# Splitting the first expert tile inside the last dense block of a fused attention, gated feed-forward and routed-experts kernel

## What is computed

```python
state = w * state + k_t v_t^T;  y_t = r_t (state + u k_t v_t^T)      # 4 x 8 heads, 768 steps, head width 48
x = (silu(x @ w_gate) * (x @ w_val)) @ w_out                         # 384 -> 1536 -> 384, every token
e = argmax(x @ moe2_w_gate)                                          # one of 8 experts for each token
out = softmax(logits)[e] * sigmoid(x @ w_output_gate)[e] * (relu(x @ w1[e]) @ w2[e])   # 384 -> 1024 -> 384
```

## Time and profile before

| | |
|---|---|
| median of 3 runs | 907.48 us (907.06 to 910.53) |
| the profiled execution: its time | 907.18 us |
| its span, first to last instruction | 905.2 us |
| mean granted TensorE clock | 0.987 of full |
| TensorE matmul busy | 859.2 us (95% of the span) |
| VectorE busy | 586.8 us (65%) |
| ScalarE busy | 300.2 us (33%) |
| GpSimd busy | 177.6 us (20%) |

### The profile page before, as it was taken

One profiled execution on the slowest core, in us unless ns is written; L12 is line 12 of the kernel. 1 busy time (PEld: TensorE's weight loads), 2 busy tenths in 40 slices (PEclk: granted clock), 3 DMA queues, 4 the chain that ended last, 5 costly groups with the idle time before them and its releaser, 6 DMA issues.

```text
span 905.2 us, 15624 instructions
## 1 busy us (share of the span) xinstructions
PE 859.2 (95%) x5725; PEld 762.4 (84%) x5725; DVE 586.8 (65%) x1075; ACT 300.2 (33%) x472; POOL 177.6 (20%) x146
## 2 busy tenths in 40 slices
PE   5799999999999999999999999997799999999996
PEld 5678888888888888888888888886799999999995
DVE  8778756675567555634443454486768777987781
ACT  1223223111311131113112312453337565665550
POOL 4823302332133312320100010130010101010110
PEclk9999999999999999999999999998899999999998
DMA  9743420242024201410010003355876668676700
GB/s 380 255 175 130 143 89 22 80 158 63 0 83 147 89 1 63 157 70 1 10 53 27 1 36 126 140 207 197 328 278 225 244 241 311 244 231 248 273 17 18
DMA packets 35934, 125.78 MB, mean 139 GB/s; under 512 B 4044, under 2 KB 19328, under 8 KB 30256
## 3 DMA queue, kind: packets, MB, share of 16 engines
q1 hardware_dynamic: 31504, 108.20, 34.5%
q0 software_dynamic: 3520, 9.87, 2.8%
q10 hardware_dynamic: 864, 7.08, 2.1%
HBM read 107.32 MB, written 18.88 MB: 139 GB/s over the span
## 4 chain that ended last, share of the span: by engine, by line
PE 84%; DVE 5%; issue 3%; DMA 3%; SPq 1%; ACT 1%; POOL 1%; DVEq 0%; ACTq 0%; POOLq 0%
PE bank L1449 33%; PE bank L1493 6%; PE bank L1495 5%; PE bank L1494 5%; PE bank L1608 4%; PE bank L1610 3%; PE bank L1609 3%; PE bank L1590 3%; PE bank L1591 3%; PE bank L1592 3%; PE bank L1374 3%; PE bank L1394 3%; PE bank L1587 2%; PE bank L1359 2%; PE bank L1386 2%
## 5 line engine op out<-in xcount | busy, mean ns | idle before, releaser
L1449 PE MATMUL bank<-X1H,WH 128*128 128x512 f32 x432 | 169.5, 392 | 4.3 <-DVE X1L L999 4.3
L1449 PE MATMUL bank<-X1H,WL 128*128 128x512 f32 x432 | 168.7, 391 | 0.0
L1449 PE MATMUL bank<-X1L,WH 128*128 128x512 f32 x432 | 168.7, 390 | 0.0
L1095 DVE TENSOR_TENSOR TT<-bank,SG 128x512 f32<-128x512 f32 x72 | 49.8, 691 | 125.0 <-ACT SG L755 124.6
L755 ACT ACTIVATE SG<-bank 128x512 f32<-128x512 f32 x72 | 43.1, 598 | 238.7 <-PE bank L1449 238.7
L686 ACT ACTIVATE AH<-PP 128x512 fp32r<-128x512 f32 (+1 forms) x78 | 46.2, 600 | 162.0 <-DVE PP L1100 162.0
L1449 PEld LDWEIGHTS bank<-X1H,WH 128*128 128x128 f32 x432 | 81.5, 189 | 21.1 <-issue 4.4
L1103 DVE TENSOR_TENSOR AL<-PP,AH 128x512 fp32r<-128x512 f32 (+1 forms) x78 | 63.2, 817 | 50.9 <-ACT AH L686 50.9
L1449 PEld LDWEIGHTS bank<-X1H,WL 128*128 128x128 f32 x432 | 81.4, 188 | 17.1
L1449 PEld LDWEIGHTS bank<-X1L,WH 128*128 128x128 f32 x432 | 81.5, 189 | 16.6
L1493 PE MATMUL bank<-AH,WH 128*128 128x512 f32 (+1 forms) x234 | 90.9, 389 | 0.0
(11 more groups left out here) (226 smaller groups left out, 1872.7 us busy)
## 6 DMA issues: line engine op xcount, KB each, us to landing
W_EVEN<-w SPq DMA_DIRECT2D x20, 1536.0 KB, 9.5
W_ODD<-w SPq DMA_DIRECT2D x18, 1536.0 KB, 9.2
RK_IN<-unit_rk SPq DMA_DIRECT2D x18, 736.0 KB, 5.5
V_IN<-unit_v SPq DMA_DIRECT2D x18, 448.0 KB, 3.7
STG<-w_dense ACTq DMA_DIRECT2D x6, 1152.0 KB, 5.4
X<-mixed SPq DMA_DIRECT2D x6, 768.0 KB, 4.4
mixed<-YS SPq DMA_DIRECT2D x40, 96.0 KB, 2.0
XG_ODD<-store SPq DMA_DIRECT2D x9, 394.0 KB, 8.4
```

What stands on the lines that cost most here:

```text
L1095: tt(TT[:, :], GATE_PS[:, :], SG[:, :], ALU.mult).then_inc(gate_free, 1)
L1449: last = mm(bank_[:, :], lhs[:, f, m, k * P:k * P + P], rhs[:, k, :], start=(x == 0), stop=(x == len(terms) - 1))
```

## The change

The high and low parts of tile 0's W1 and rows, and the high parts of its W2, are made inside the last dense block (W1 at f = 9 and 10, rows at f = 10 after a `turn_rows` on PE placed there, W2 highs at f = 10 and 11). The first two slices of tile 0's up product run ahead of the last down product, the others behind it. To have the PSUM banks free for that, the hidden banks are taken in the order 5, 0, 1, 6. PAD is filled in the block at f = 6, and the early tiles are chosen at f = 4 (two) and f = 5. SP loads tile 2 right behind W1 of tile 1, ahead of the pad stores. POOL's slice of W1 low is now one of tile 1, not of tile 0. The tail of the last block is put between the steps of tile 0 in a new order on each engine: on DVE the low parts of tile 1's W1 and rows and gates(0) are made ahead of positions(CH); on PE ranks(CH) and the turning of tile 1's rows are between the two halves of tile 0's down product. Functions that only moved up in the file are left out of the diff.

```diff
-        H_PS, XT_PS, YO_PS = (bank[0], bank[1], bank[5], bank[6]), (bank[7], bank[4]), bank[2:4]
+        H_PS, XT_PS, YO_PS = (bank[5], bank[0], bank[1], bank[6]), (bank[7], bank[4]), bank[2:4]
...
+            load_tile(EARLY_TILES[2], early_row(2), early_expert(2))
 
             sp.wait_ge(base_ready, 1)
+            sp.wait_ge(padding, 2)
             sp.nop(nofuse=True)
             for x in range(NE):
                 row = sp.value_load(BASEI[0:1, x:x + 1], min_val=x * REGION, max_val=x * REGION + TOK)
                 sp.dma_start(store[bass.ds(row, SLOT), :].rearrange("(a p) c -> p a c", p=P), PAD[:, :, :])\
                   .then_inc(pad_written, 16)
-            load_tile(EARLY_TILES[2], early_row(2), early_expert(2))
 
...
-            pool.wait_ge(w1_high, 2)
+            tile = EARLY_TILES[1]
+            pool.wait_ge(w1_high, 3 * tile.n + 2)
+            pool.wait_ge(w1_low, 3 * tile.n)
             cut = slice(EF, 2 * EF)
-            nc.gpsimd.tensor_tensor(W1L[0][:, cut], W1[0][:, cut], W1H[0][:, cut], ALU.subtract).then_inc(w1_low, 1)
+            nc.gpsimd.tensor_tensor(W1L[1][:, cut], W1[1][:, cut], W1H[1][:, cut], ALU.subtract).then_inc(w1_low, 1)
...
+                    if last and f == 9:
+                        w1_highs(EARLY_TILES[0])
+                    if last and f == 10:
+                        x_highs(EARLY_TILES[0])
+                        w2_highs(EARLY_TILES[0], 0)
+                    if last and f == 11:
+                        w2_highs(EARLY_TILES[0], 1)
...
-                    if isinstance(tile.n, int) and tile.n == 0:
-                        if f % 2 == 0:
-                            w2_highs(tile, f // 2)
-                    elif next_tile and f < KT:
+                    if next_tile and f < KT:
                         w1_highs(next_tile, range(f, f + 1))
                 if next_tile:
                     act.wait_ge(hidden_ready, 4 * tile.n + 4)
                     x_highs(next_tile)
-                    if isinstance(tile.n, int) and tile.n == 0:
-                        w1_highs(next_tile)
                     w2_highs(next_tile, 0)
                     w2_highs(next_tile, 1)
 
-            act.wait_ge(value_ready, FT * CH)
-            w1_highs(EARLY_TILES[0])
+            dense_block(0)
+            with act.Fori(1, CH - 1) as n:
+                dense_block(n)
+            dense_block(CH - 1)
+
+            tile, following = EARLY_TILES[0], EARLY_TILES[1]
+            hidden_highs(tile, 0)
             x2_copies(CH)
-            x_highs(EARLY_TILES[0])
+            hidden_highs(tile, 1)
             rec_copies(CH)
-            act.wait_ge(x2_ready, KT * CH)
-
-            expert_tile(EARLY_TILES[0], EARLY_TILES[1])
+            hidden_highs(tile, 2)
+            hidden_highs(tile, 3)
+            w1_highs(following)
+            exps(tile)
+            x_highs(following)
+            w2_highs(following, 0)
+            w2_highs(following, 1)
...
+            def fill_pad():
+                for x in range(2):
+                    dve.wait_ge(y_stored[x], 64 * CH - 64)
+                dve.wait_ge(r_scaled, UNITS)
+                nc.vector.memset(PAD[:, :, :], 0.0).then_inc(padding, 1)
+                dve.wait_ge(padding, 1)
+                for x in range(2):
+                    last = nc.vector.tensor_scalar(PAD[:, x, R_ID:R_ID + 1], CST[:, C_TOK:C_TOK + 1], float(TOK + x * P),
+                                                   None, ALU.add)
+                last.then_inc(padding, 1)
...
-                        if last and f in (4, 5, 6):
-                            choose_early(f - 4)
+                        if last and f == 4:
+                            choose_early(0)
+                            choose_early(1)
+                        if last and f == 5:
+                            choose_early(2)
+                        if last and f == 6:
+                            fill_pad()
+                        if last and f == 9:
+                            w1_lows(EARLY_TILES[0], (0, 1))
+                        if last and f == 10:
+                            w1_lows(EARLY_TILES[0], (2,))
+                            x_lows(EARLY_TILES[0])
...
-            for x in range(2):
-                dve.wait_ge(y_stored[x], 64 * CH - 64)
-            dve.wait_ge(r_scaled, UNITS)
-            c = Chain(setup, c.at + c.k)
-            c.step(nc.vector.memset(PAD[:, :, :], 0.0))
-            for x in range(2):
-                c.step(nc.vector.tensor_scalar(PAD[:, x, R_ID:R_ID + 1], CST[:, C_TOK:C_TOK + 1], float(TOK + x * P), None,
...
-            w1_lows(EARLY_TILES[0], (0,))
-            x2_copy(CH)
-            w1_lows(EARLY_TILES[0], (2,))
-            x_lows(EARLY_TILES[0])
-            rec_copy(CH)
-            copy_logits(CH)
-            gates(EARLY_TILES[0])
-            route(CH)
-            copy_ranks(CH)
-            positions(CH)
-            nc.vector.tensor_copy(BASEI[:, :], BASE[:, :]).then_inc(base_ready, 1)
...
-                first = isinstance(tile.n, int) and tile.n == 0
-                if not first:
-                    gates(tile)
+                gates(tile)
                 if tile.half_tile:
                     sum_halves(tile, 0)
                     sum_halves(tile, 1)
@@ -1251,23 +1259,38 @@
                     hidden_lows(tile, f)
                     if tile.half_tile and f < 2:
                         sum_halves(tile, f + 2)
-                    if first:
-                        if f % 2 == 0:
-                            w2_lows(tile, f // 2)
-                    elif next_tile and f < KT:
+                    if next_tile and f < KT:
                         w1_lows(next_tile, range(f, f + 1))
                     if isinstance(tile.n, int) and tile.n == 1:
                         (plan_counts, plan_kinds, plan_entries, plan_rows)[f](plan)
                 if next_tile:
                     x_lows(next_tile)
-                    if first:
-                        w1_lows(next_tile)
                     w2_lows(next_tile, 0)
                     w2_lows(next_tile, 1)
                 scale_rows(tile)
 
-            dve.wait_ge(x2_ready, KT * CH)
-            expert_tile(EARLY_TILES[0], EARLY_TILES[1])
+            tile, following = EARLY_TILES[0], EARLY_TILES[1]
+            dve.wait_ge(down_done, (FT - 1) * CH)
+            w2_lows(tile, 0)
+            hidden_lows(tile, 0)
+            x2_copy(CH)
+            hidden_lows(tile, 1)
+            rec_copy(CH)
+            w2_lows(tile, 1)
+            hidden_lows(tile, 2)
+            copy_logits(CH)
+            hidden_lows(tile, 3)
+            w1_lows(following, (0,))
+            route(CH)
+            copy_ranks(CH)
+            w1_lows(following, (2,))
+            x_lows(following)
+            gates(tile)
+            positions(CH)
+            nc.vector.tensor_copy(BASEI[:, :], BASE[:, :]).then_inc(base_ready, 1)
+            w2_lows(following, 0)
+            w2_lows(following, 1)
+            scale_rows(tile)
...
+            def expert_down(tile, halves=None):
+                wh, wl = W2H[tile.buffer], W2L[tile.buffer]
+                need(pe, yo_scaled, tile.before)
+                for half in halves or tile.halves:
...
+                    if last and f == FT - 2:
+                        pe.wait_ge(y_added, UNITS)
+                        pe.wait_ge(ranks_copied, CH - 1)
+                        turn_rows(EARLY_TILES[0])
                     if f >= 1:
                         down(n, f - 1)
+                if last:
+                    expert_up(EARLY_TILES[0], range(0, 2))
                 down(n, FT - 1)
...
-            pe.wait_ge(y_added, UNITS)
-            pe.wait_ge(ranks_copied, CH - 1)
...
-            turn_rows(EARLY_TILES[0])
+            tile = EARLY_TILES[0]
+            pe.wait_ge(gate_free, FT * CH)
+            pe.wait_ge(value_free, FT * CH)
+            expert_up(tile, range(2, 4))
             turn(CH)
-            expert_up(EARLY_TILES[0], range(0, 1))
+            expert_up(tile, range(4, 6))
             route_logits(CH)
-            expert_up(EARLY_TILES[0], range(1, 2))
+            expert_up(tile, range(6, ET))
             turn_logits(CH)
-            expert_up(EARLY_TILES[0], range(2, 4))
-            ranks(CH)
-            expert_up(EARLY_TILES[0], range(4, ET))
-            pe.wait_ge(logits_read, CH)
-            pe.wait_ge(ranks_copied, CH)
             pe.wait_ge(rec_act, 2 * CH)
             pe.wait_ge(rec_dve, CH)
+            expert_down(tile, [0])
+            pe.wait_ge(logits_read, CH)
+            ranks(CH)
+            pe.wait_ge(ranks_copied, CH)
             turn_rows(EARLY_TILES[1])
-            expert_down(EARLY_TILES[0])
+            expert_down(tile, [1])
 
```

More of the change, by code:

```diff
@@ L375, in rwkv_moe_moe @@
         plan_ready = sem("plan_ready")
+        padding = sem("padding")
         pad_written = sem("pad_written")
@@ L738, in dense_block @@
                 first = isinstance(n, int) and n == 0
```

(53 more changed lines are left out.)

97 lines of the change are left out of this document (45 added, 52 removed).

## The result

The changed kernel takes 900.44 us as the median of 7 runs (898.56 to 902.6); the kernel before took 905.27 us in the 7 runs that go with it (904.56 to 910.53). The ratio is 0.9924 with a 95% interval of 0.9907 to 0.9941: 6.9 us of 905.27, between 5.3 and 8.4. The two medians alone lie only 4.8 us apart, less than that interval has; the 7 runs of before are three at 907.06 to 910.53 and four at 904.56 to 905.27, so their median is a loose measure. The comparison was repeated later, 6 runs of the changed kernel against 11 of before, with medians of 901.04 and 907.50 (6.5 us apart) and a ratio of 0.9925 (0.9900 to 0.9951). The profiled execution took 899.33 us, its span is 897.5. So it is faster, as forecast, and by both ratios by more than the 4.9 us of my sum (0.54%).

The account below looks back on a forecast made before the run. VectorE's plan, late through SP's queue order, was taken to bound the kernel. Removing VectorE's 6.30 us wait, less a 1.4 us later tail, gave 4.9 us: 907.18 to 902.3, or 902.6 from the median; range 898.5 to 906.5.

Parts of the forecast that it names:

- What bounds the kernel: Everything behind 650 us hangs on VectorE finishing the plan; tile 3's rows land 15.4 us after it.
- The cause of the biggest hole: SP's queue: eight pad stores ahead of tile 2's weights made VectorE stand still 6.30 us and TensorE wait 6.6 us.
- The work moved into the dense block: Early splitting in the last dense block's steps of f costs nothing, up to 2.5 us a step.
- VectorE's chain by its new order: Tail on VectorE up to HL ends 1.4 us later, but without the 6.30 us wait: 620.8 becomes 615.9, 4.9 us earlier.
- The held EQ: In VectorE's route, EQ waits for GpSimd's W1 low until 602.2; priced between 0 and 1.9 us, taken at 1.9.
- The size: Whole kernel 4.9 us faster: 907.18 us becomes 902.3, or 902.6 from the median.
- is no term of the sum by itself: TensorE's 2.37 us tail hole counts only as far as it brings VectorE's chain forward; TensorE waits for tile 3's rows anyway.
- Everything behind shifts by 4.9 us: After tile 3's rows the hole stays some 5 us with half clock behind it; all later work moves 4.9 us earlier.
- Small instructions not held: Rival: GpSimd does not hold VectorE's small routing instructions; chain gains the whole 1.9 us, plan at 627.9, 900.4 us; chance 0.20.
- W1 of tile 1 as the wait: Rival: tile 1's W1, issued 2.7 us later, arrives late for ScalarE; 3.2 of the 4.9 us go, 905.5; chance 0.12.
- The change does not reach the plan: Rival: TensorE's holes near 585 to 600 stay under other names; 0 to 3 us come through, about 905.7; chance 0.10.
- The clock: Rival: TensorE pauses between 617 and 626 bring half clock through down(1) and up(2); 2.7 us slower, 909.9; chance 0.08.

Follow-up runs that it names:

- e5_plan_ahead: Changed kernel with VectorE's four plan parts directly behind tile 1's hidden lows, tile 2's three W1 lows behind the plan; 897.08 us, ratio to before 0.9867.
- e1_sp_order_only: Kernel before with one edit: SP loads tile 2 ahead of the eight pad stores; 901.23 us against 907.87, ratio 0.9928.
- e2_pads_first: Changed kernel with SP loading tile 2 behind the pad stores again, early splitting kept; 919.97 us, ratio to before 1.0136.
- e8_rows_first: Changed kernel with SP asking for tile 3's rows ahead of its W1 and W2; 895.78 us, ratio to before 0.9866.
- e0_after_again: Changed kernel run once more, unaltered; 901.04 us, ratio to before 0.9925.
- e7_order_and_plan: Kernel before with tile 2 loaded ahead of the pads and the plan ahead of tile 2's W1 lows on VectorE; 898.59 us, ratio 0.9886.
- e3_no_gpsimd_slice: Changed kernel with GpSimd's slice of tile 1's W1 low made by VectorE instead; 899.85 us, ratio to before 0.9925.

## Why the prediction was right, and where it was wrong

**What bounds the kernel: right.** VectorE's plan, through SP's wait for it and the flight of tile 3's rows, sets the end of the stretch. e5_plan_ahead moved the plan by 3.40 us and the landing by 3.06 (there SP's last wait ahead of tile 3's loads is for the pads and no longer for STI, and its first load follows STI's end by 2.5 us in place of 1.8). From STI's end to landed rows it took 15.1 us, forecast 15.4. The pads did not become a wait in the changed kernel.

**The cause of the biggest hole: right.** It was SP's order. e1_sp_order_only and e2_pads_first show it from both sides.

**The work moved into the dense block: right,** it cost nothing: TT of f = 9 to TT of f = 11 is 12.94 us (566.52 to 579.46), 12.24 before, and the difference of 0.70 is about the six transposes (0.66), which the sum had.

**VectorE's chain by its new order: right to 0.3 us** by that profile, in part by luck. Counted from the anchor, tile 2's first W1 low was forecast at 615.9 less 567.95, 47.95; it came at 614.20 less 566.52, 47.68. The held EQ, which I priced between 0 and 1.9 and took at 1.9, took 1.70 more than its 0.19 us. The other value would have been wrong by nearly the whole of it; the nearest row, a large subtraction, told of a small one correctly. The luck is the clock: 0.5 us of the 47.68 is the half clock behind the hole ahead of the ranks, for which the sum had nothing. With full clock there (e8_rows_first) the same W1 low comes at 47.16, 0.8 ahead of the forecast. The hole itself, 1.6 us and 0.5 more behind it, was not forecast either; by the sum's own reasoning it costs only TensorE time that is otherwise spent waiting for tile 3's rows.

**The size: too small.** The sum had 4.9 us; the ratio says 6.9 (5.3 to 8.4), the medians of the repeat 6.5. Only the medians of the first 7 runs, 4.8 apart, would meet the forecast. Two steps of the sum failed.

The first is the sentence that the tail's 2.37 us hole on TensorE "is no term of the sum by itself": the clock behind the hole was put at nothing. In the profile that I had, full clock followed the hole. In the second profile of before, half clock did, and the plan was 1.2 us later from the anchor. The change takes this hole away, so it also takes away a cost that I could not see in the one execution that I had, and that the second profile of before paid. What it puts in its place, the hole ahead of the ranks, costs 0.5 us of plan when half clock follows. Against the second profile the plan gains 6.1 to 6.4 us (67.69 less 61.58 or 61.33). The Trainium skill, page "TensorE: Matmul & The Clock Gate", section "Part 1: The HAM clock gate (the "warmup" mystery)", says that the place where the clock rises at the start of a kernel varies between runs of the same kernel; these two profiles show the like in mid-kernel, 0.60 and 1.00 in the same stretch.

The second is "Everything behind shifts by 4.9 us". From the landed rows to the end it took 255.2 and 256.3 us before and 254.4 and 254.3 after: 0.8 to 2.0 us more gained behind the rows, which my sum had at nothing. It divides into two parts. From the landing to the first wait of the late loop it is 36.9 and 37.2 us before and 36.7 in both profiles after: 0.2 to 0.5 us, because the half clock behind the rows ends sooner (granted clock in 649 to 653: 0.50 in both before, 1.00 in both after). The other 0.7 to 1.6 us is in the six late passes, 3 and 6 long ones against 1 and 1. Since variants of the changed kernel have 2 to 5 long ones, this part is not shown to be the change's.

Together, in the mean of two profiles each: the landing is 5.7 us earlier, the first wait of the late loop 6.1 (119.5 less 113.5), the end 7.1 (338.28 less 331.14). In the profiles that the sum is measured by, the landing came 5.4 us earlier: 0.3 more than forecast by VectorE's chain and 0.3 by the way from plan to landing (15.1 for 15.4). The rest up to the late loop, 0.6 us in these means, goes with the clock: half clock behind the tail's hole in one of the two profiles of before, and longer behind the rows in both. Whether the last microsecond, that of the passes, belongs to the change stays open.

**The rivals.** Small instructions not held: fell. W1 of tile 1 as the wait: fell, ScalarE began it at once behind its fourth HH, and SP had issued it at 587.18. The change does not reach the plan: fell. The clock: TensorE did pause in down(1), 3.2 us in two waits, and half clock followed (0.62 in 625 to 629):

```profile
625.00:629.00 4.00, 4.00 (x16) 4.00 (x16) 3.79 (x13) 0.00 (x0) 0.20 (x1) 0.62 0.12 49
```

but it was over by 633, and TensorE still came 3.4 us ahead of the rows. In e0_after_again the same two waits (3.1 us) were followed by full clock, and TensorE came 5.3 us ahead.

## What to carry to other kernels

When a wait on a busy engine ends with a DMA, read the issuing queue first: here eight stores that nobody needed for another 25 us stood ahead of the load that everybody waited for, and one moved line was worth the whole rewrite around it; with a second small edit on VectorE's order (e7_order_and_plan) it was worth more. An edit's showy part (early splitting, products ahead of others) may bring nothing, and be a loss without the plain one; undo the parts singly. One profile shows one course of TensorE's clock; price each short hole on TensorE in both courses, and compare stretches from a common instruction rather than by whole times when the start scatters.

## What the runs showed of the hardware that I had not expected

- A 2.35 to 2.37 us hole on TensorE, in the same program at the same place, was followed by full clock in one execution and by half clock in another (1.00 and 0.60 of 590 to 594). The same holds of longer ones: the 3.4 us hole for tile 3's rows in the changed kernel was followed by half clock (0.60 in 644 to 647), the 3.5 us one in e3_no_gpsimd_slice was not (1.00 in 644 to 647). Where half clock followed, the way from the landing to the late loop took 36.6 to 37.2 us, where it did not (e3, e5, e7) 35.2.
- The beginning of the program scatters by 4.6 us between profiles (first TT at 50.2 to 54.8), nearly as much as the change moves the plan (5.2); the part from there to the anchor takes 515.6 to 516.6 us in each.
- A 128x32 VectorE instruction with two SBUF operands was held 1.7 us by a GpSimd subtraction that had begun 0.6 us before it, while the copy and the reduction between the two were not. The Trainium skill, page "SBUF — State Buffer", section "Who interferes with whom", says that a VectorE instruction with two SBUF inputs contends with a GpSimd instruction that reads SBUF, that the shared ports are locked exclusively, and that issue order decides who blocks. The runs agree: EQ ended 0.05 us after GpSimd, and was back at 0.19 us without the slice.
